# A sliding-window attention and mixer kernel: q and k of sequences 1 to 3 turned in 32x32 blocks by VectorE instead of transposed by TensorE

## What is computed

```python
scores = scale * np.matmul(q, k.transpose(0, 1, 3, 2))
rel = pos[:, None] - pos[None, :]
mask = (rel >= 0) & (rel < window)                 # window = 64
attn = softmax(np.where(mask, scores, -1000000000.0))
x = np.matmul(attn, v)                             # heads side by side: (B, S, 512)
h = np.maximum(x @ w_in, 0.0); u, v = h[..., :512], h[..., 512:]
v_s = np.einsum('ts,bsd->btd', w_spatial, norm(v)) + b_spatial
x = (u * v_s) @ w_out
h = np.maximum(xt @ w_tok1, 0.0) @ w_tok2          # xt = x transposed: over tokens
u = x + h.transpose(0, 2, 1)
out = u + np.maximum(u @ w_ch1, 0.0) @ w_ch2
```

## Time and profile before

| | us |
|---|---|
| median of 3 runs | 735.2 (734.97 to 735.63) |
| the profiled execution | 734.2 |
| its span, first to last instruction | 732.1 |
| stage of sequence 1, 2 | 99.2, 94.9 |
| TensorE busy | 699.1 (95% of the span) |
| VectorE, ScalarE, GpSimd busy | 292.2, 259.8, 153.0 |
| mean granted TensorE clock | 0.988 of full speed |

### The profile page before, as it was taken

One profiled execution on the slowest core, in us unless ns is written; L12 is line 12 of the kernel. 1 busy time (PEld: TensorE's weight loads), 2 busy tenths in 40 slices (PEclk: granted clock), 3 DMA queues, 4 the chain that ended last, 5 costly groups with the idle time before them and its releaser, 6 DMA issues.

```text
span 732.1 us, 11665 instructions
## 1 busy us (share of the span) xinstructions
PE 699.1 (95%) x4313; PEld 646.4 (88%) x4313; DVE 292.2 (40%) x812; ACT 259.8 (35%) x693; POOL 153.0 (21%) x237
## 2 busy tenths in 40 slices
PE   5799899999999999999999689999999999999998
PEld 5688898989998899989998689999989999998997
DVE  4975964663637547365382312111121121121110
ACT  5566356433556335563336212111211221211211
POOL 3731525430234311163146220000000000000000
PEclk9999999999999999999999989999999999999999
DMA  7761312122221303003430400020110200200101
GB/s 161 225 160 30 90 44 51 36 73 47 51 46 26 95 18 70 22 2 112 148 108 1 169 27 0 2 86 1 46 40 0 86 0 0 87 1 0 44 1 43
DMA packets 70368, 41.21 MB, mean 56 GB/s; under 512 B 57264, under 2 KB 60912, under 8 KB 70320
## 3 DMA queue, kind: packets, MB, share of 16 engines
q1 hardware_dynamic: 70320, 40.56, 19.7%
HBM read 31.11 MB, written 9.44 MB: 55 GB/s over the span
## 4 chain that ended last, share of the span: by engine, by line
PE 92%; DVE 4%; issue 1%; POOL 1%; DMA 1%; ACT 1%; SPq 0%; POOLq 0%; DVEq 0%; ACTq 0%
PE ps L1024 66%; PE ps L1115 11%; PE ps L1084 4%; PE ps L1059 4%; PE ps L1043 2%; PE ps L1069 2%; PE ps L1178 1%; PE ps L1257 1%; DMA att<-in_moe_w_ch_dram 1%; DVE att L828 1%; DVE den L837 0%; POOL att L576 0%; DVE arena L939 0%; DVE att L810 0%; DVE att L808 0%
## 5 line engine op out<-in xcount | busy, mean ns | idle before, releaser
L1024 PE MATMUL ps<-arena 128*128 128x288 f32 (+3 forms) x2064 | 363.5, 329 | 10.2 <-DVE att_r L999 7.2
L1024 PEld LDWEIGHTS ps<-arena 128*128 128x128 f32 (+1 forms) x2064 | 326.6, 188 | 28.4 <-DVE att_r L999 7.4
L1024 PE MATMUL ps<-arena,att_r 128*128 128x512 f32 x648 | 161.2, 393 | 0.0
L999 DVE SCALAR_TENSOR_TENSOR att_r<-ps,att_r 128x384 fp32r<-128x384 f32 x72 | 40.1, 558 | 257.7 <-ACT att_r L770 257.7
L1024 PEld LDWEIGHTS ps<-arena,att_r 128*128 128x128 f32 x648 | 120.7, 188 | 21.9
L770 ACT ACTIVATE att_r<-ps 128x384 fp32r<-128x384 f32 x72 | 35.3, 491 | 247.8 <-PE ps L1024 247.8
L1115 PE MATMUL ps<-arena 128*128 128x288 f32 (+1 forms) x560 | 100.0, 325 | 5.9 <-DVE arena L939 5.9
L1115 PEld LDWEIGHTS ps<-arena 128*128 128x128 f32 x560 | 81.2, 190 | 10.4 <-DVE arena L939 7.1
L576 POOL TENSOR_SCALAR att<-att,rinv 128x128 f32<-128x128 f32 x144 | 57.3, 416 | 138.6 <-DVE rinv L839 138.3
L652 ACT ACTIVATE att<-att,nmax 128x128 f32<-128x128 f32 x144 | 56.0, 390 | 22.4 <-DVE nmax L828 22.2
L1059 PE MATMUL ps<-att 128*128 128x128 f32 x288 | 40.5, 289 | 1.6 <-DVE att L817 1.6
(11 more groups left out here) (76 smaller groups left out, 505.9 us busy)
## 6 DMA issues: line engine op xcount, KB each, us to landing
u_scratch<-uy SPq DMA_DIRECT2D x16, 288.0 KB, 2.2
out_dram<-att SPq DMA_DIRECT2D x18, 256.0 KB, 2.1
att<-in_q_dram SPq DMA_DIRECT2D x16, 256.0 KB, 3.3
att<-in_k_dram SPq DMA_DIRECT2D x16, 256.0 KB, 3.2
att<-in_v_dram SPq DMA_DIRECT2D x16, 256.0 KB, 3.2
att<-in_moe_w_ch_dram SPq DMA_DIRECT2D x8, 384.0 KB, 5.6
att<-in_moe_w_ch_dram SPq DMA_DIRECT2D x6, 512.0 KB, 4.3
xT<-u_scratch SPq DMA_DIRECT2D x3, 768.0 KB, 4.7
```

Source lines behind the costliest of these rows:

```text
L999: dve.scalar_tensor_tensor(out=h3[:, j % RING, 1, :], in0=ps[:, 6 + j % 2, 0:CK], scalar=0.0, in1=h3[:, j % RING, 0, :].bitcast(F32), op0= ...
L1024: ins = pe.matmul(dst, w[a], x[c], start=first and n == 0, stop=last and n == 2, skip_group_check=True)
```

## The change

For sequences 1 to 3 a sequence's q and k are loaded in thirds of 192 tokens. `load_third` issues 16 DMAs for a third of q or of k: for each pair of heads, each head of it and each half of its 64 numbers, 32 partitions (the token within a group of 32) x 6 groups x 32 numbers. A piece of 32 numbers is 128 bytes in a row of memory; before it was 64 numbers, 256 bytes. The thirds lie in the old room of the tiles, one buffer for q and one for k, and a third is loaded once the one before it has been turned. VectorE turns them in blocks of 32x32: `q_turn` (qt0 to qt8, one for each block of 64 tokens, two instructions) writes into `qd`, whose room is now cut by blocks, and `k_turn` (kt0 to kt2, one for each third, one instruction) into `kT`. S waits for the turns. Q, K, Z, qe, ke and ze of these sequences are gone, and the tables of all engines are written in another order; the prologue and the epilogue of TensorE, and the arithmetic, are as before. Sequence 0 is transposed by TensorE as before.

```diff
+            def load_third(kind, b, x):
+                s, src = (0, q) if kind == "lq" else (1, k)
+                if (b, x) == (1, 0):
+                    sp.wait_ge(*use_full(*(("K", 0, NT - 2) if s == 0 else ("Z", 0, NT - 1))))
+                else:
+                    b0, x0 = divmod(3 * (b - 1) + x - 1, 3)
+                    sp.wait_ge(turned, TURNED[("qt", b0 + 1, PER_THIRD * x0 + PER_THIRD - 1) if s == 0 else ("kt", b0 + 1, x0)])
+                for w in range(PAIRS):
+                    for h in range(2):
+                        for g in range(2):
+                            c = D * h + 32 * g
+                            sp.dma_start(third[c:c + 32, s, w * THIRD:(w + 1) * THIRD].rearrange("p (i d) -> p i d", d=32),
+                                         src[b, 2 * w + h, x * THIRD:(x + 1) * THIRD, 32 * g:32 * g + 32]
+                                         .rearrange("(i p) d -> p i d", p=32)).then_inc(third_in[s], 16)
...
+            def q_turn(b, blk):
+                g = BL * b + blk
+                at = blk % PER_THIRD * WINDOW
+                dve.wait_ge(third_in[0], 16 * 16 * (3 * (b - 1) + blk // PER_THIRD + 1))
+                apart(dve)
+                dve.wait_ge(sc_full, g - 3)
+                for h in range(2):
+                    c = slice(h * D, (h + 1) * D)
+                    ins = dve.transpose(qd[c, g // 2 % 2, g % 2, :, h, :],
+                                        third[c, 0, :].rearrange("p (w n) -> p w n", w=PAIRS)[:, :, at:at + WINDOW])
+                ins.then_inc(turned, 1)
+
+            def k_turn(b, x):
+                dve.wait_ge(third_in[1], 16 * 16 * (3 * (b - 1) + x + 1))
+                apart(dve)
+                dve.wait_ge(sc_full, BL * (b - 1) + min(PER_THIRD * (x + 1), BL - 1) + 1)
+                dve.transpose(kT[:, :, x * THIRD:(x + 1) * THIRD], third[:, 1, :].rearrange("p (w n) -> p w n", w=PAIRS)) \
+                    .then_inc(turned, 1)
...
-                if t < NT - 1:
+                if b > 0:
+                    pe.wait_ge(turned, max(TURNED["qt", b, blk], TURNED["kt", b, blk // PER_THIRD]))
+                elif t < NT - 1:
...
     LOOP_PE = (
-        "g00 Q0 + K0 g10 Q1 + g20 K1 + S0 g30 S1 + g01 Q2 + g11 T0 + K2 g21 V0 + g31 T1 + S2 y00 + V1 y10 + S3 "
+        "g00 S0 + S1 g10 + S2 g20 + g30 + g01 T0 T1 + S3 g11 + S4 g21 + g31 + y00 V0 V1 + T2 y10 + V2 y20 + T3 "
```

More of the change, by code:

```diff
@@ L38, in bass_attention_gmlp_mixer_kernel @@
     WINS = BL - 1
+    THIRD = S // 3
+    PER_THIRD = THIRD // WINDOW
     SCALE = float(D) ** -0.5
@@ L60, in bass_attention_gmlp_mixer_kernel @@
     FIRST_PE = (
[3 rows of a table removed]
-        "u30 + u01 + u11 + u21 + u31 +").split()
+        "g00 + g10 + g20 S0 + S1 g30 + S2 g01 + g11 + g21 + g31 T0 + T1 y00 V0 S3 S4 + V1 T2 y10 + S5 y20 + V2 "
+        "y30 + y01 T3 S6 T4 S7 V3 V4 + y11 + y21 + y31 + t0 t1 T5 T6 S8 a0 t2 a1 t3 V5 V6 a2 t4 a3 T7 a4 T8 V7 V8 "
+        "b00 b10 b20 b30 b01 b11 b21 b31 v0 + v1 + v2 + v3 + v4 + u00 + u10 + u20 + u30 + u01 + u11 + u21 + u31 +").split()
     LOOP_PE = (
[3 rows of a table removed]
-        "u30 + u01 + u11 + u21 + u31 +").split()
[3 rows of a table added]
+        "u31 +").split()
     EPILOGUE_PE = (
@@ L76, in bass_attention_gmlp_mixer_kernel @@
     FIRST_ACT = (
[L77 to L79 removed]
+        "gh00 gh10 gh20 e0 e1 gh30 e2 gh01 gh11 o0 e3 yy00 e4 yy10 o1 e5 yy20 gh21 gh31 yy30 o2 e6 e7 o3 o4 yy01 "
+        "yy11 yy21 yy31 th0 th1 e8 th2 th3 o5 o6 th4 ah0 ah1 o7 o8 vr0 vr1 vh0 vr2 vh1 vr3 vh2 vr4 uu00 vh3 uu10 "
+        "uu20 vh4 uu30 uu01 uu11 uu21 uu31").split()
     LOOP_ACT = (
[L81 to L83 removed]
+        "e0 gh00 e1 gh10 e2 gh20 gh30 gh01 e3 gh11 e4 o0 o1 yy00 gh21 gh31 yy10 o2 yy20 yy30 o3 yy01 yy11 o4 yy21 "
+        "yy31 e5 th0 th1 e6 e7 th2 th3 e8 th4 o5 o6 ah0 ah1 o7 vr0 o8 vr1 vh0 vr2 vh1 vr3 vh2 vr4 uu00 vh3 uu10 "
+        "uu20 vh4 uu30 uu01 uu11 uu21 uu31").split()
     EPILOGUE_ACT = (
@@ L106, in bass_attention_gmlp_mixer_kernel @@
     FIRST_POOL = (
-        "lo0 lo1 lo2 lo3 la0 la1 la2 n0 n1 n2 n3 lb0 lb1 xh0 xh1 xl0 xl1 n4 n5 n6 n7 xh2 xl2 n8 xh3 rs0 xl3 rs1 "
-        "xh4 xl4 rs2 rs3 rs4").split()
+        "lo0 lo1 lo2 lo3 n0 n1 n2 la0 la1 la2 n3 n4 lb0 lb1 n5 n6 n7 xh0 xh1 xl0 xl1 n8 xh2 xl2 xh3 xl3 xh4 xl4 "
+        "rs0 rs1 rs2 rs3 rs4").split()
     LOOP_POOL = (
-        "n0 n1 n2 n3 xh0 xh1 xl0 xl1 n4 n5 n6 n7 xh2 xl2 n8 xh3 rs0 xl3 rs1 xh4 xl4 rs2 rs3 rs4").split()
+        "n0 n1 n2 n3 n4 xh0 xh1 xl0 xl1 n5 n6 n7 n8 xh2 xl2 xh3 xl3 rs0 xh4 xl4 rs1 rs2 rs3 rs4").split()
     EPILOGUE_POOL = (
@@ L223, in bass_attention_gmlp_mixer_kernel @@
         nat = room("nat").rearrange("p (s n) -> p s n", s=3)
+        third = room("nat").rearrange("p (s n) -> p s n", s=2)
         pT = room("pT").rearrange("p (s n) -> p s n", s=2)
@@ L311, in bass_attention_gmlp_mixer_kernel @@
         tp_dve = sem("tp_dve")
+        turned = sem("turned")
+        third_in = [sem("third_in_q"), sem("third_in_k")]
         sc_full = sem("sc_full")
@@ L358, in bass_attention_gmlp_mixer_kernel @@
         TP_DVE = counts(DVE_ORDER, ("ke", "c"))
+        TURNED = counts(DVE_ORDER, ("qt", "kt"))
         PIECE_HI = counts(DVE_ORDER, ("hv", "hu", "ho", "ha", "hb"))
@@ L451, in _ @@
         def _(sp):
+            def load_third(kind, b, x):
[12 more added lines that the diff above has]
+                                         .rearrange("(i p) d -> p i d", p=32)).then_inc(third_in[s], 16)
             def load(kind, b, x):
-                if kind in ("lq", "lk", "lz"):
+                if kind in ("lq", "lk") and b > 0:
+                    load_third(kind, b, x)
+                elif kind in ("lq", "lk", "lz"):
                     e = nat_entry("K" if kind == "lk" else "Q", b, x)
@@ L959, in _ @@
                     k_out(b, x)
+                elif kind == "qt":
+                    q_turn(b, x)
+                elif kind == "kt":
+                    k_turn(b, x)
                 elif kind == "vo":
```

16 lines of the change are left out of this document (4 added, 12 removed), and 26 rows, old and new, of tables (ALL_SP, FIRST_DVE, FIRST_PE, LOOP_DVE).

## The result

The changed kernel takes **756.6 us** (median of 4 runs, 753.7 to 758.4) against 735.1 for the kernel before beside it: a ratio of 1.030, with an interval of 1.027 to 1.032. It is slower by 21.5 us. The prediction said slower by 50, 785.4 us, with a range of 746 to 815. The sign and the mechanism came out, the size did not.

A forecast was written before the change was run, and what follows sets the result against it. TensorE, busy 95% of the span, was taken as the bound, with SyncE's issues deciding the change: 40.9 + 4.8 + 4.5 = 50.2 us on 734.2 gives 784.4, plus 1.0 for the median: 785.4 us, range 746 to 815.

The forecast's parts named there:

- The bound of half a copy: VectorE's turns, bounded from below by a copy inside SBUF, 512 numbers in 0.42 us: about half the forecast cost.
- that of twice: VectorE's turns, bounded from above at twice the forecast cost, since no trace row excludes it.
- the first wait: TensorE in sequences 2 and 3: waits first at S3, for the middle third of q.
- the 16 us of waits forecast up to V2: TensorE in sequences 2 and 3: 16 us of waits in all, at S3, V0 and V2; V2 wanted at 25.6, ready at 41.7.
- the rival of short issues: SyncE: issues at most 0.39 us from start to start, V2 in time, 728 us; 5 in 100.
- the pair of 64 partitions: SyncE's trace row of a 64-partition DMA following another: 0.634 us an issue, 0.65 from start to start; 0.64 was taken.
- the run of seven: SyncE's trace row of seven large DMAs in a run: 3.40 / 7 = 0.49 us an issue.
- the bounds, 0.41 to 0.77: SyncE, us per issue: 0.367 plus a 0.04 gap below; 0.65 plus half the step from 0.41 to 0.65 above.
- in a run of large DMAs or between, p 0.41 to 0.52: SyncE: p is us from issue start to issue start; 746 us at 0.47, 739 at 0.41; 17 in 100.
- the first rival: SyncE: issues hidden by the DMAs themselves, at most 0.39 us each, so 728 us; 5 in 100.
- my terms for a0, clock and small waits: Sequences 1 to 3: later a0 +14.3, +15.4, +11.2 us; clock falls 4.8 and small waits 4.5 in all.
- the paper gain of 13.8: TensorE: 9.7 us of transpositions, 2.5 of a wait in sequence 1 and 1.6 of slow clock gone.

The follow-up runs named there:

- the run on shapes: Changed kernel plus bursts of four DMAs of each of eight shapes at the end of SyncE's queue, into unused rooms; 796.8 us in one run.

## Why the prediction was right in kind and wrong in size

**Right.** TensorE loses 108 matmuls. The turns cost 0.87 and 0.98 us where 0.86 and 0.95 were worked out from passes of other kinds over as many numbers in the earlier trace rows; the figure that I had put beside them from the Trainium skill (VectorE: DVE Perf Modes, "The three transpose paths") is for bf16 and 128x128, which no run here has. The bound of half a copy and that of twice are both out. The waits stand at S, V and a0 in front of VectorE, with a DMA ahead of VectorE's turns and SyncE's queue ahead of the DMA, as the steps had it; the chain names SyncE's issue line for 14%. One place was wrong: in sequences 2 and 3 nothing waits ahead of S3, where the first wait was forecast. Of the 16 us of waits forecast up to V2 there, 4.8 came in sequence 2 (3.29 and 1.50). With the loads gone the kernel takes 728.8 us, and the rival of short issues had been priced at 728, by giving back "about half" of the gain, which was a judgement.

**Wrong: the price of an issue.** The step that failed is this term of the sum. It was taken as 0.64 us from start to start and is 0.48, or 0.51 with its pauses; the landing was taken as 3.2 us and is 1.9. 16 thirds of 16 issues on the path x (0.64 − 0.51) = 33 us, and 3 x 1.3 = 4 us of landings: that is more than the miss of 28.8. What went wrong in it is the choice between rows. I took the pair of 64 partitions as "nearest in shape" and left the run of seven, at 0.49 the other row for issues in a long run, to the rival. The measured value lies inside the bounds, 0.41 to 0.77, and inside the rival "in a run of large DMAs or between, p 0.41 to 0.52", which had 17 in 100 and 746 us. Behind the choice stood a rule that I had read into two rows, 128 partitions cheap and 64 dear: fewer partitions, dearer. Two rows that differ in more than the partitions cannot show it, and the run on shapes shows that it isn't so.

The Trainium skill (DMA: Bandwidth & Descriptors, "Issuing engines are not separate DMA queues") says that the time to initiate a DMA is usually small against the DMA. For this kernel the trace disagrees: one issue of 0.44 us is a quarter of the 1.9 us to landing, but sixteen of them are 7.7 to 9 us against 1.9, and it is the issues that the end waited for. By that rule the kernel would have come to the first rival's 728 us, and 756.6 was measured.

**Wrong the other way: what the corrected sum leaves out.** With 0.51 and 1.9 put in, the sum gives 785.4 − 37 = 748, and 756.6 was measured. By sequence, against the corrected sum (my terms for a0, clock and small waits less 96, 96 and 64 issues of 0.13 us and one landing each), the stages should be 3.6, 4.7 and 4.7 us longer, and are 7.7, 6.6 and 4.9. So the forecast would have been 8 to 9 us too low with the right price: the two errors have opposite signs, and the second hides a part of the first. Sequence 1 has the largest part: the load of w_tok's piece was counted as one issue more, and what it waits for was not; it held the queue for 4.1 us, and moving it gave 5.4 (735.4 to 730.0). The prediction should have asked of each entry of that table not only how long its issue is but until when it may not start. The rest, some 2 us in sequence 2, has not been taken apart.

**The small terms.** The clock was to cost 4.8 us. It is 0.979 on the mean, 0.988 before. In the three stages it was 0.95, 0.98 and 0.98, where the earlier trace rows has 0.98 and 1.00: if nothing of it fell into idle time this is 0.03 x 107 + 0.02 x 101 + 0.02 x 100 = 7.2 us at most. The window in which the wait of 3.29 us in sequence 2 ends shows the clock down (0.57 on its mean, most of it near the half level), and one 4 us later shows it back at full (the third number from the end):

```profile
208.00:212.00 4.00, 3.60 (x18) 3.63 (x19) 1.35 (x6) 0.91 (x4) 2.54 (x8) 0.57 0.31 50
216.00:218.00 2.00, 1.77 (x14) 1.77 (x15) 1.33 (x4) 0.86 (x4) 0.00 (x0) 1.00 0.33 52
```

With all of that the sum is waits 28.4 − 7.4 = +21.0, transpositions −9.7, the clock at most +7.2: +18.5, and the spans differ by 19.5. What of the clock's part is real no run here separates. The removed wait of 2.46 us in sequence 1 did not leave nothing: waits of 1.13 and 1.83 us stand in its place, with or without the loads, the first for a q turn and the second for a maximum that VectorE makes behind two q turns and a cast. These two, and 2.07 for 1.65 us at a0, are a part of what the paper gain of 13.8 had forgotten.
